# Constant products of TensorE in the two gaps of each routing step and ahead of the first step

## The reference

```python
x = attention(q, k, v)          # 2 x 8 heads, 768 positions, window 128 + 4 sinks -> 1536 tokens x 512
logits = x @ w_gate             # 1536 x 8 experts
order = np.argsort(-logits.flatten())
for idx in order:               # greedy, best pair first; each expert takes cap = 192 tokens
    tok, e = idx // 8, idx % 8
    if assigned[tok] >= 0 or counts[e] >= cap: continue
    assigned[tok] = e; counts[e] += 1
out[mask_e] = relu(x[mask_e] @ w1[e]) @ w2[e]     # for each expert e, D = 512, F = 1024
y = (out @ w_a) * (out @ w_b) @ w_out             # 512 -> 1536 -> 512
```

## Time and profile before

| | us |
|---|---|
| time, median of 3 runs | 621.92 (621.45 to 622.95) |
| the profiled execution's own time | 623.54 |
| its span, first to last instruction | 621.8 |
| TensorE busy | 583.5 (94%) |
| VectorE busy | 416.4 (67%) |
| ScalarE busy | 316.0 (51%) |
| GpSimd busy | 337.5 (54%) |

### The profile page before, as it was taken

The page is one execution under the profiler, slowest core; times in us unless marked ns, Lnnn a source line. Parts: engine busy times, 40 slices in busy tenths (PEclk is TensorE's granted clock), DMA queues, the critical chain, the costliest instruction groups (busy, mean ns, idle before and its releaser), DMA issues.

```text
span 621.8 us, 11131 instructions
## 1 busy us (share of the span) xinstructions
PE 583.5 (94%) x3820; PEld 526.8 (85%) x3820; DVE 416.4 (67%) x1079; ACT 316.0 (51%) x766; POOL 337.5 (54%) x408
## 2 busy tenths in 40 slices
PE   8999999994359999999999999999999999999996
PEld 4888778863229999999999999999999999999984
DVE  3789669847844776767986566747746646656663
ACT  3788669742205766768775445433534424424410
POOL 6211101110012512267886999997997898687623
PEclk9999999996559999999999999999999999999999
DMA  9995060405012776667662222313222322210102
GB/s 189 273 198 126 20 187 27 162 27 162 1 53 69 251 219 223 205 208 248 221 207 100 74 96 69 102 37 100 69 67 69 119 86 101 67 47 23 34 1 101
DMA packets 87674, 72.12 MB, mean 116 GB/s; under 512 B 40000, under 2 KB 74816, under 8 KB 87616
## 3 DMA queue, kind: packets, MB, share of 16 engines
q1 hardware_dynamic: 83888, 64.64, 35.3%
q0 software_dynamic: 1920, 6.29, 3.0%
q10 hardware_dynamic: 1808, 0.44, 0.4%
HBM read 65.08 MB, written 6.29 MB: 115 GB/s over the span
## 4 chain that ended last, share of the span: by engine, by line
PE 81%; DVE 10%; POOL 4%; ACT 2%; issue 2%; ACTq 1%; DVEq 0%; POOLq 0%
PE psum L1885 12%; PE psum L1964 9%; PE psum L1967 9%; PE psum L1966 9%; PE psum L1886 6%; PE psum L1879 5%; PE psum L1880 5%; PE psum L1687 5%; PE psum L1878 5%; PE psum L1649 4%; PE psum L1670 3%; PE psum L1626 2%; DVE above L1339 2%; DVE w_lo L1102 1%; POOL x_hl L743 1%
## 5 line engine op out<-in xcount | busy, mean ns | idle before, releaser
L779 POOL TENSOR_TENSOR w_lo<-w_raw,w_hi 128x512 fp32r<-128x512 f32 x96 | 109.6, 1174 | 24.1 <-ACT w_hi L995 24.1
L1885 PE MATMUL psum<-h_hl,w_hi 128*128 128x384 f32 x256 | 75.8, 364 | 0.6 <-POOL w_lo L702 0.6
L1885 PE MATMUL psum<-x_hl,w_hi 128*128 128x384 f32 x256 | 74.3, 362 | 0.3 <-DVE x_hl L1474 0.3
L1966 PE MATMUL psum<-x_hl,w_hi 128*128 128x384 f32 x216 | 72.2, 334 | 0.0
L862 ACT ACTIVATE w_hi<-w_raw 128x1024 fp32r<-128x1024 f32 (+1 forms) x72 | 69.1, 960 | 0.0
L1102 DVE TENSOR_TENSOR w_lo<-w_raw,w_hi 128x1024 fp32r<-128x1024 f32 x44 | 65.1, 1480 | 0.0
L1886 PE MATMUL psum<-x_hl,w_lo 128*128 128x192 f32 x256 | 64.3, 251 | 0.0
L1886 PE MATMUL psum<-h_hl,w_lo 128*128 128x192 f32 x256 | 64.2, 251 | 0.0
L1602 DVE TENSOR_TENSOR o_acc<-psum,o_acc 128x512 f32<-128x512 f32 x60 | 41.2, 690 | 34.2 <-PE psum L1880 34.0
L687 POOL CAST p_sink<-p_sb 128x16 fp32r<-128x16 f32 x40 | 8.1, 204 | 99.0 <-ACT p_sb L883 78.6
L1964 PE MATMUL psum<-x_hl,w_hi 128*128 128x384 f32 x168 | 56.3, 335 | 0.4 <-POOL w_lo L779 0.4
(11 more groups left out here) (236 smaller groups left out, 1529.8 us busy)
## 6 DMA issues: line engine op xcount, KB each, us to landing
w_raw<-in_moe_w_dram SPq DMA_DIRECT2D x32, 1024.0 KB, 5.5
w_raw<-in_moe_w_a_dram SPq DMA_DIRECT2D x12, 512.0 KB, 3.6
w_raw<-in_moe_w_b_dram SPq DMA_DIRECT2D x12, 512.0 KB, 3.6
w_raw<-in_moe_w_out_dram SPq DMA_DIRECT2D x12, 512.0 KB
k_raw<-in_k_dram SPq DMA_DIRECT2D x16, 192.0 KB, 4.3
v_sb<-in_v_dram SPq DMA_DIRECT2D x16, 192.0 KB, 4.3
xs_scratch<-x_rows SPq DMA_DIRECT2D x8, 384.0 KB, 3.5
q_raw<-in_q_dram SPq DMA_DIRECT2D x14, 192.0 KB, 4.4
```

The source lines that it names most:

```text
L779: return nc.gpsimd.tensor_tensor(out_t, t, hi_t.bitcast(f32), ALU.subtract)
L1885: nc.tensor.matmul(bk[:, 0:2 * CAP], lhs_hi, rhs_both, start=first, stop=False)
L1966: nc.tensor.matmul(o, w_h, t_lo[:, t, :], start=False, stop=False, skip_group_check=True)
```

## The change

One wait and four products ahead of the first step; four products between the counts of the constant and the first wait for `above` in each of the 7 steps; five behind the products of the scales and the lift in each of the first 6.

```diff
             last.then_inc(gate_ready, 1)
+            pe.wait_ge(x_kept, STEPS_A)
+            spinning(4, bank[6])
             for st in range(STEPS):
                 pe.wait_ge(oh_ready, st + 1)
                 for c in range(OWN, NCH):
 
                     nc.tensor.matmul(bank[1][:, 0:E], ones16[:], oh[:, c, :], start=(c == OWN), stop=False)
+                spinning(4, bank[6])
                 for no in range(HALVED):
                     pe.wait_ge(above_ready, HALVED * st + no + 1)
...
                     for zone, by in enumerate((scale_by[:, 0, :], scale_by[:, 1, :], lift_by[:])):
                         last = nc.tensor.matmul(bank[4][:, zone * E:(zone + 1) * E], by, full[:], start=True, stop=True)
                     last.then_inc(scales_ready, 1)
+                    spinning(5, bank[6])
             def positions():
```

## The result

The changed kernel takes 624.51 us (median of 11 runs, 623.55 to 625.69) where the kernel before takes 622.59 (median of 11 beside it). The ratio is 1.0034, with a 95% interval of 1.0025 to 1.0043: 2.1 us slower (1.6 to 2.7). The forecast was 621.2 us and no measurable change, the range ended at 624.0 us. The forecast started from 621.92 us, the median of three runs; beside the changed kernel the kernel before has 0.67 us more, so 0.7 of the 3.3 us between forecast and result are that starting point and not the change.

A forecast was written before the change was run, and what follows sets the result against it. The prediction took VectorE's chain, not TensorE, to bound the routing steps. Gains of 0.56 in passages and 0.2 in positions, less 0.1, made about 0.7 us off the 621.92 us median: 621.2 us, range 619.9 to 624.0 us.

The forecast's parts named there:

- the products fit at the high level: Ahead of step 0 and in both gaps, 0.2 to 0.3 us stay left; the 62 added products cost 0.
- the shift of 0.76 us: Behind the routing, the twelve constant products start 0.76 us earlier, stay at 0.42 us each and pass the shift on.
- The gain per passage: Two TensorE passages in each of 7 steps get 0.04 us shorter each at the high level, 0.56 us in all.
- The 0.2 us in the positions: Behind the steps, the eleven L1814 products save about 0.2 us if the high level still holds.
- The level holds: Granted clock 1.00 from 144 to 173 us; the forecast, level held and little gained, had chance 0.55.
- The rival of the swinging clock: In the steps, a low level costs 0.65 us per step; three of six low steps give 623.4 us; chance 0.25.
- The sum: Whole kernel: 0.56 + 0.2 - 0.1 = 0.66, say 0.7 us gained, giving 621.2 us.

The follow-up runs named there:

- the second repeat: The changed kernel run once more, unchanged, for another profile, in which the level fell at 160.3 us; 625.35 us in a single run.
- the two repeats: The changed kernel run twice more, unchanged, for further profiles; 624.55 and 625.35 us, single runs.
- the kernel with five and six: Changed kernel with 5 and 6 constant products in the gaps instead of 4 and 5, plus 53 of 8 columns behind the steps; ratio 1.0000 to the kernel before.
- the kernel with 62 small products: Kernel before plus the change's wait and 62 products in the same places, each 8 columns wide instead of 512; ratio 1.0028 to the kernel before.
- 24 small products: Kernel before with 24 products of 8 columns added behind the last step; ratio 1.0017 to the kernel before.
- four kernels: Change plus 66 small products; gaps of five and six; streaming in the first gap only; gaps of three and four: ratios 1.0009, 1.0000, 1.0013, 1.0000 to the kernel before.

## Why the prediction was wrong

*That the products fit at the high level and cost nothing there.* Right for TensorE's time in the gaps: steps of 4.21 us, TensorE never late at 1.00. Ahead of step 0 the level was not the high one (low from 142.7 to 146.1 us), so that the counts came at 144.92 instead of 144.12 us; TensorE caught up in the profiled execution, and lost 0.26 us there in the second repeat. Wrong as a statement on the added work. The sentence "At the high level all three places have 0.2 to 0.3 us left: the cover is VectorE's own chain, and the added work costs 0" priced 62 products by streaming alone. They are also 124 more instructions that TensorE must be fed, a weight load and a product each, and with them the last fetch came behind the start of the branch instead of ahead of it. This is the step that failed. It cost 1.1 us of branch in the profiled execution and 1.4 in the two repeats; 62 products of 8 columns alone cost 1.7 us of time. The prediction had the place in view ("issue" of 2.12 us ahead of L1621 in the earlier trace rows) and did not ask what it was.

*That the branch and the twelve products would follow the shift of 0.76 us.* With the fetch moved, they came 1.19 us later instead.

*The gain per passage, 0.04 us between bounds of 0.002 and 1.8/14 = 0.13.* Measured 0.01: (4.23 - 4.21)/2. The lower end, which came from the duration of the small products themselves (180 against 186 ns), was the right neighbour; the difference of the 512-column products was not. The steps brought 0.12 us, not 0.56. From VectorE's copy of the last logits (L1315) to the token lists (`ids`, L1464) are 36.20 us before:

```profile
143.24 0.21 DVE L1315 COPY L<-psum 128x48 f32<-128x48 f32 x1 [1.65 <-PE psum L1785]
...
179.44 0.17 DVE L1464 TENSOR_TENSOR ids<-psum,id_lane 128x12 int32<-128x12 f32 x1
```

and 36.08 us in the changed kernel:

```profile
143.44 0.21 DVE L1315 COPY L<-psum 128x48 f32<-128x48 f32 x1 [1.85 <-PE psum L1785]
...
179.52 0.17 DVE L1464 TENSOR_TENSOR ids<-psum,id_lane 128x12 int32<-128x12 f32 x1
```

L1806, the sum over the partitions, in the changed kernel:

```profile
L1806 PE MATMUL psum<-full,ones x7: 179/180/189, 147.2 to 172.4; 128*128 128x8 bf16 x7
```

*The 0.2 us in the positions.* None: the level had fallen at 170.0 us, and the eleven products took 0.47 us as before. In the kernel with five and six it held until 173.6 us.

*The level holds.* Half right. It was low under step 0, held over most steps and fell again, at 170.0 us in the profiled execution and in mid-routing in both repeats. The rival of the swinging clock had the mechanism: at the low level the two gaps overrun together, by 0.58 and 0.29 us where 0.65 was worked out, and the first gap alone costs the steps nothing. It had too many spells, three low steps where each repeat shows one spell among the later steps. The fuller gaps of five and six held the level from 147 us on, the kernel's 4 and 5 didn't always. The Trainium skill ("TensorE: Matmul & The Clock Gate", section "A second HAM failure mode: psum-queue depth-cycling") says that short idle times between groups can make the clock swing; the traces agree, with one spell among the steps at 157.1 and one at 160.3 us.

*The sum.* From the logits' copy to the first expert product the three profiles of the changed kernel have 46.32, 47.26 and 47.04 us, the kernel before 45.33. That is +1.0, +1.9 and +1.7 us, against 2.1 us measured. In the two repeats 0.44 us of it lies in the routing and 1.3 to 1.5 us from the token lists to the experts. The clock rival's 623.4 us lies nearest to the 624.51 measured, but by luck: it holds 2.0 us for low steps, where the repeats lost 0.58 and 0.55 us in them, and nothing for the branch. The times of the kernel with 62 small products (1.7 us more, 1.1 to 2.4) and of the change (2.1, 1.6 to 2.7) overlap, so how the rest is shared between clock and branch is not settled by them.

A part of the scatter belongs to neither kernel. From the first expert product to the start of the last product of all, the profiles have either 425.7 to 426.0 us (ten of the fourteen, the changed kernel's first among them) or 426.5 to 426.7 us (before, the one with 62 small products, five and six, one repeat). In the profiled pair, whose first expert products start 1.19 us apart, this took back 0.8 us, which is why the two spans, 621.8 and 622.2 us, show so little of the loss. What makes the difference was not tried.

## What to carry to other kernels

Count added instructions as well as added work: ahead of a branch that skips its body, instructions that cost no time of their own can move an instruction fetch to the wrong side of the branch. Look at "issue" time at a branch before and after, and pad or move instructions to tell where the fetch falls from what the edit does, before blaming or praising the edit. A shorter branch is no shorter kernel by itself: with 24 small products it fell from 2.32 to 0.36 us, and the median time did not fall. Before filling gaps to hold the clock, ask what the products on the path gain by it: here they have 8 columns, and 28 us mostly at the doubled clock were worth 0.12 us, while a fill sized for the high level overran when the level dropped. A path of wider products was not tried.

## What had not been expected of the hardware

The instruction fetches of q8 are of 16384 bytes and begin up to 28 us apart. The branch over the body lasted 0.36 to 0.37 us in the four profiles in which the last fetch ahead of it had begun 4.9 to 5.3 us earlier. In the ten others it lasted 1.23 to 3.76 us and ended 2.45 to 2.88 us after the start of a fetch. The length doesn't depend on the count of instructions alone: with 128 products added it was 2.14, 2.34, 2.52 and 1.59 us in four kernels whose added products stand in different places, which also changes when the fetch begins.
